# Other step numbers for the side work of a fused attention and MLP kernel

## The reference

```python
# attention without a softmax of q.k: q and k each get a softmax of their own
q_s = exp(q - max(q, -1)); q_s = q_s / (sum(q_s, -1) + 1e-9)
k_s = exp(k - max(k, over tokens)); k_s = k_s / (sum(k_s, over tokens) + 1e-9)
kv  = einsum('bhsd,bhse->bhde', k_s, v)
x   = einsum('bhsd,bhde->bhse', q_s, kv)      # then (B*S, 512)
# first MLP
h = x @ w_in; g = relu(h) ** 2; x = g @ w_out      # 512 -> 2048 -> 512
# second MLP
xn = x / sqrt(mean(x*x) + 1e-6) * rms_g
out = (silu(xn @ w_gate) * (xn @ w_val)) @ w_out   # 512 -> 1536 -> 512
```

## Time and profile before

| | |
|---|---|
| median of 3 runs | 1646.05 us |
| the profiled execution | 1645.26 us, of which the span is 1643.0 us |
| granted clock of TensorE | 1.000 |
| PE busy | 1627.4 us (99%) |
| DVE busy | 1175.4 us (72%) |
| ACT busy | 646.0 us (39%) |
| POOL busy | 584.6 us (36%) |

### The profile page before, as it was taken

One profiled execution on the slowest core, in us unless ns is written; L12 is line 12 of the kernel. 1 busy time (PEld: TensorE's weight loads), 2 busy tenths in 40 slices (PEclk: granted clock), 3 DMA queues, 4 the chain that ended last, 5 costly groups with the idle time before them and its releaser, 6 DMA issues.

```text
span 1643.0 us, 26962 instructions
## 1 busy us (share of the span) xinstructions
PE 1627.4 (99%) x10106; PEld 1479.0 (90%) x10106; DVE 1175.4 (72%) x1808; ACT 646.0 (39%) x1224; POOL 584.6 (36%) x467
## 2 busy tenths in 40 slices
PE   7999999999999999999999999999999999999999
PEld 6999999999988888888888989988988989999999
DVE  7798778777667778887867565556556568877785
ACT  6565445543323333333334423333333345433442
POOL 3563332333002225522338654555555552000000
PEclk9999999999999999999999999999999999999999
DMA  8676545654643344343442223241331245443441
GB/s 277 198 253 206 173 164 180 202 176 144 221 144 111 107 159 126 117 127 117 128 128 83 104 90 136 69 142 64 110 103 64 100 138 169 160 148 131 140 141 52
DMA packets 149505, 230.09 MB, mean 140 GB/s; under 512 B 11392, under 2 KB 73600, under 8 KB 149376
## 3 DMA queue, kind: packets, MB, share of 16 engines
q1 hardware_dynamic: 149376, 228.37, 42.0%
HBM read 143.39 MB, written 84.93 MB: 139 GB/s over the span
## 4 chain that ended last, share of the span: by engine, by line
PE 91%; DVE 3%; DMA 2%; POOL 2%; issue 1%; ACT 1%; SPq 0%; DVEq 0%; ACTq 0%; POOLq 0%
PE bank L1957 16%; PE bank L1959 16%; PE bank L1958 16%; PE bank L2043 8%; PE bank L2045 8%; PE bank L2044 8%; PE bank L2132 5%; PE bank L2134 5%; PE bank L2133 5%; PE bank L1950 2%; PE bank L1927 1%; DMA araw<-a_scratch 1%; DVE OA L1742 0%; DMA SA<-in_s 0%; PE bank L1978 0%
## 5 line engine op out<-in xcount | busy, mean ns | idle before, releaser
L1957 PE MATMUL bank<-TR,SW 128*128 128x512 f32 (+1 forms) x840 | 308.6, 367 | 0.3 <-DVE TR L1662 0.3
L1959 PE MATMUL bank<-TR,SW 128*128 128x512 f32 (+1 forms) x840 | 308.7, 368 | 0.0
L1958 PE MATMUL bank<-TR,SW 128*128 128x512 f32 (+1 forms) x840 | 308.6, 367 | 0.0
L1957 PE MATMUL bank<-TAR,SA 128*128 128x288 f32 x784 | 244.4, 312 | 1.4 <-issue 1.4
L1958 PE MATMUL bank<-TAR,SA 128*128 128x288 f32 x784 | 231.2, 295 | 0.0
L1959 PE MATMUL bank<-TAR,SA 128*128 128x288 f32 x784 | 230.5, 294 | 0.0
L2045 PE MATMUL bank<-GH,W 128*128 128x512 f32 x576 | 224.2, 389 | 0.0
L2044 PE MATMUL bank<-GH,W 128*128 128x512 f32 x576 | 224.2, 389 | 0.0
L2043 PE MATMUL bank<-GH,W 128*128 128x512 f32 x576 | 224.1, 389 | 0.0
L1226 ACT ACTIVATE GH<-g 128x512 fp32r<-128x512 f32 x144 | 91.1, 634 | 241.3 <-DVE g L1562 162.8
L2132 PE MATMUL bank<-SW,OA 128*128 128x256 f32 x630 | 178.3, 283 | 0.0
(11 more groups left out here) (179 smaller groups left out, 3299.9 us busy)
## 6 DMA issues: line engine op xcount, KB each, us to landing
h_scratch<-hb SPq DMA_DIRECT2D x128, 288.0 KB, 2.8
hst<-h_scratch SPq DMA_DIRECT2D x144, 256.0 KB, 2.7
araw<-a_scratch SPq DMA_DIRECT2D x18, 1536.0 KB, 6.8
...
```

What stands on the lines that cost most here:

```text
L1957: nc.tensor.matmul(ps[:, 0:w], w_hi[:, cc], x_hi[:, c], start=opens and c == 0, stop=False, skip_group_check=True)
L1958: nc.tensor.matmul(ps[:, 0:w], w_lo[:, cc], x_hi[:, c], start=False, stop=False, skip_group_check=True)
L1959: last = nc.tensor.matmul(ps[:, 0:w], w_hi[:, cc], x_lo[:, c], start=False, stop=c == 1, skip_group_check=True)
```

## The change

Only numbers of the tables are changed: the steps at which pieces of side work are put into the queues. No instruction is added or taken away. Nearly half of the entries move, most by one or two steps. The core of the diff:

```diff
-UNIT_PE = [("KM", (6, 19, 31, 39), (3, 15, 26, 34)),
+UNIT_PE = [("KM", (7, 21, 29, 39), (4, 15, 26, 35)),
...
-UNIT_DVE = [("qmax", (1, 11, 21, 32), (-3, 3, 16, 23)),
-            ("kmax", (3, 6, 26, 34), (-3, 5, 22, 31)),
+UNIT_DVE = [("qmax", (-6, 11, 21, 32), (-4, 2, 16, 23)),
+            ("kmax", (5, 13, 25, 35), (0, 7, 21, 32)),
...
-add_batches(POOL_AT, "sum", [(T1, 29), (T2, 46), (T3, 51), (T4, 54)], [], [])
+add_batches(POOL_AT, "sum", [(T1, 31), (T2, 42), (T3, 47), (T4, 48)], [], [])
```

More of the change, by code:

```diff
@@ L108 @@
 ALONE_BANKS = 6
-UNIT_PE = [("KM", (6, 19, 31, 39), (3, 15, 26, 34)),
[3 rows of a table removed]
-UNIT_DVE = [("qmax", (1, 11, 21, 32), (-3, 3, 16, 23)),
-            ("kmax", (3, 6, 26, 34), (-3, 5, 22, 31)),
[L118 to L131, removed]
+UNIT_PE = [("KM", (7, 21, 29, 39), (4, 15, 26, 35)),
[3 rows of a table added]
+UNIT_DVE = [("qmax", (-6, 11, 21, 32), (-4, 2, 16, 23)),
+            ("kmax", (5, 13, 25, 35), (0, 7, 21, 32)),
+            ("qmax2", (4, 15, 24, 35), (-3, 9, 19, 28)),
+            ("qsum", (7, 18, 27, 38), (4, 12, 24, 37)),
+            ("qinv", (9, 22, 30, 41), (5, 15, 26, 38)),
+            ("readKM", (9, 22, 31, 41), (4, 16, 25, 37)),
+            ("qturn", (14, 25, 34, 44), (11, 16, 28, 39)),
+            ("readKV", (17, 27, 37, 47), (12, 19, 31, 42))]
+UNIT_ACT = [("qmaxswap", (3, 13, 23, 34), (-4, 6, 18, 24)),
+            ("qexp", (4, 16, 27, 37), (1, 12, 23, 33)),
+            ("qsumswap", (8, 20, 29, 40), (5, 15, 25, 37)),
+            ("kexp", (12, 24, 34, 42), (7, 16, 28, 40)),
+            ("readX0", (20, 30, 44, 49), (16, 25, 34, 44)),
+            ("readX1", (22, 33, 48, 51), (17, 30, 38, 47))]
+UNIT_POOL = [("qsub", (3, 11, 25, 35), (0, 10, 21, 32)),
+             ("qnorm", (6, 23, 30, 43), (6, 15, 27, 38))]
 UNIT_SP = [("q", (-15, 1, 13, 23), (-12, -8, 8, 14)),
[1 row of a table removed]
[1 row of a table added]
            ("kt", (-5, 5, 16, 27), (-9, 0, 11, 22)),
@@ L154, in add_batches @@
             table.setdefault(start_of(b) + n - STEPS, []).append((what, b, i))
-add_batches(ACT_AT, "split", [(B11, 25), (T1, 49), (T2, 50), (B21, 51), (T3, 54), (T4, 56)], [(B22, 63)], [(B22, 63)])
-add_batches(DVE_AT, "split", [(B11, 30), (T1, 50), (T2, 50), (B21, 51), (T3, 57), (T4, 57)], [(B22, 64)], [(B22, 64)])
-add_batches(POOL_AT, "sum", [(T1, 29), (T2, 46), (T3, 51), (T4, 54)], [], [])
+add_batches(ACT_AT, "split", [(B11, 25), (T1, 50), (T2, 50), (B21, 50), (T3, 56), (T4, 56)], [(B22, 61)], [(B22, 64)])
+add_batches(DVE_AT, "split", [(B11, 28), (T1, 50), (T2, 50), (B21, 51), (T3, 57), (T4, 57)], [(B22, 64)], [(B22, 64)])
+add_batches(POOL_AT, "sum", [(T1, 31), (T2, 42), (T3, 47), (T4, 48)], [], [])
 for _m in range(2, PA):
```

## The result

The changed kernel takes 1658.53 us (median of 4, 1658.16 to 1659.42), the kernel before, run beside it, 1645.82 us (median of 4): 1.0077 times the time, 95% interval 1.0058 to 1.0094. It is slower, by 12.7 us, where 7.9 were forecast, and 0.5 us above the top of the range. The profiled execution took 1658.94 us with a span of 1656.8 (before: 1645.26 and 1643.0).

The account below looks back on a forecast made before the run. TensorE, busy 99% of the span, was taken as the bound, so only its pauses count. Blocks 2 to 6 (5.9), block 1 (2.3) and the plain part (-0.3) add 7.9 us: forecast 1653.7 us, range 1645.0 to 1658.0.

Parts of the forecast that it names:

- KM of unit 2: Round in blocks 1 to 6: the swap now stands ahead of the `readX0` it needs; wait of 0.47 us each.
- Blocks 2 to 6: Five blocks with the same orders: each 1.18 us longer from waits and restarts, 5.9 us together.
- Step 10: Group 1's B21 in blocks 2 to 6: waits for `h_copy_p1` behind two swaps, 0.35 plus restart 0.07, 0.42 us.
- step 9: Group 1's T1 in blocks 2 to 6: waits for VectorE's later `h_12`, 0.27 plus restart 0.07, 0.34 us.
- The start of a block: Blocks 2 to 6: `h_12` comes 0.11 us later, but step 3 waits no more; together -0.05 us.
- Moved rounds: X0, X1 and KM behind other TensorE steps: taken as nothing, bounds -0.4 to +0.4 us over 6 blocks.
- Block 1: Step 10 there comes late behind splits and two swaps, 1.82 us, plus 0.47 for KM: 2.3 us.
- the case slower still: Rival: other places late too, such as GpSimd's weight sums beside block 1 and the plain part; 1657 or more, chance 0.12.
- The plain part: Stretch where batch 1's steps move: few waits seen, taken as -0.3 us, bounds -0.7 to +1.8.
- Faster (kmax the whole wait): Rival at block starts: the merge doesn't hold VectorE up, step 2 never waits; 1642 us, chance 0.12.
- The case of no change: Rival: VectorE and ScalarE are ahead enough that the waits of steps 9 and 10 vanish; 1646 to 1649, chance 0.16.
- The price of a swap: ScalarE's four small copies: 0.90 us by the trace, 1.26 by the skill's budget, which gives 1662; chance 0.02.

Follow-up runs that it names:

- after_swap9: The changed kernel with ScalarE's swap of unit 1 put back at step 9, behind `h_copy_p1` of group 1: 1653.68 us.
- after_read24: The changed kernel with ScalarE's read of X0 of unit 1 put back at step 24, ahead of the swap of unit 3: 1656.17 us.
- before_kmax0: The kernel before with one entry changed, `kmax` of unit 0 in the later batches moved from -3 to 0: 1647.54 us.
- first_old: The changed kernel with all entries of the first batch (the plain part) as before: 1654.44 us.
- after_s14: The changed kernel with GpSimd's sums of chunk 4 (s1) three steps later, away from VectorE's splits in block 1: 1657.33 us.
- plain_dve: The changed kernel with only VectorE's first-batch entries as before: 1661.90 us, plain part 66.99.
- plain_rest: The kernel before with only VectorE's first-batch entries as changed: 1647.88 us, plain part 61.86.

## Why the prediction was wrong in size and right in kind

- *Slower, and by the mechanism named:* right. Steps 9 and 10, KM of unit 2 behind a swap, the pause of 0.61 ahead of the merge, TensorE's work unchanged.
- *Blocks 2 to 6, 5.9:* measured 6.2. Step 10 0.42 (0.40 by after_swap9), KM 0.47 (0.49 by after_read24), step 9 0.34 (0.18 + 0.10 in the trace, 0.24 by before_kmax0). The start of a block -0.05: TensorE stands 0.06 better at step 4 and 0.03 at step 8, but over another path: step 1 waits 0.26 for `h_21`, which I let pass although my own walk put it behind `qmax`. Moved rounds 0 +-0.4: 0.11 to 0.14 per block, 0.6 to 0.7 in five and outside my bounds. I had taken TensorE's side alone; the round that came a step earlier meets its operand (X0 and `bd`, 0.12). That the sum is right to 0.06 per block is in part luck: step 9 was 0.06 too dear and the rounds 0.11 too cheap.
- *Block 1, 2.3:* this term was mis-sized, 3.67. The step that failed is the walk's "the splits 88.65, `qmax` 89.99": I took the 1.34 of a block in which GpSimd is idle. Beside its sums they took 2.51, and 0.5 more is waited at step 6. I had named these sums in the case slower still and given them no number. With the splits at 1.42 (first_old) the walk to step 12 holds, 1.78 for 1.82; the longer splits add 1.07, the moved rounds 0.1, and KM costs 0.73 in this block for 0.47. That the gain at step 10 is given back at KM (after_s14) says that this block has more than one late chain.
- *The plain part, -0.3, bounds -0.7 to +1.8:* this is the step that failed most, 2.7 of the 6.0 us of span by which the forecast was short (block 1 1.4, the start 1.35, blocks 2 to 6 0.3, behind them 0.3); without any one of the first three the time would have been inside the range. Measured +2.38, and between +1.1 and +3.3 in the seven kernels with these entries. I bounded it by one added wait, since rows at hand showed one; the first-batch entries of all five engines move by up to 7 steps, and the trace after has several waits in it. I walked a block exactly and a longer stretch not at all. Which of these waits comes from which entry stays open; plain_dve and plain_rest put the loss on the entries of the engines other than VectorE, SyncE among them.
- *The start:* 1.35 us net, 1.60 by TensorE's clock, no term of mine. Without the 1.35 the profiled execution would stand at 1657.6.
- *The rivals.* Faster (kmax the whole wait) fell in before_kmax0: the swap holds step 3. The case of no change fell with the waits at steps 9 and 10, which are there. Slower still (1657 or more; the plain part at its upper bound and one wait in block 1) is what happened, at 0.12 against 0.60. Its range should have been wider upwards: it was the case with the unwalked terms.
- *The price of a swap:* 0.90 for four copies in every chain after, as in the earlier trace rows. The Trainium skill's budget (ScalarE: Activation LUTs, Rules for kernel authors) would have it at 1.26 by my estimate; the trace does not agree.

How far single parts can be read: the same entries gave

| part | kernels with the same entries | lowest to highest, us |
|---|---|---|
| plain part, before's entries | 8 | 60.9 to 61.8 |
| plain part, changed entries | 7 | 62.2 to 64.5 |
| block 1, before's entries | 3 | 51.3 to 53.0 |
| all behind block 7 | 18 | 1193.9 to 1196.3 |
| blocks 2 to 6, within one kernel | 5 each | at most 0.03 apart |

So differences in blocks 2 to 6 are good to some 0.03 us, and those under 1.5 us in the other two are not shown by one profile's length; there only the single waits, read step by step, say where a part was lost. The 1196.3 is first_old's, whose profiled execution is 1.7 us above its median.
